# Waits, one store and the width of the output matmuls in a delta-rule attention and MLP kernel

## The reference

```python
k_n = k / (np.linalg.norm(k, axis=-1, keepdims=True) + 1e-06)
for t in range(S):
    y[:, :, t] = q_t @ state                  # per batch and head, state is D x D
    state = state + bt * outer(k_t, v_t - state.T @ k_t)
x = y.transpose(0, 2, 1, 3).reshape(B * S, H * D)          # 3072 x 384
x = ((x @ w1) * (x @ w2) @ w3) @ w_out                     # 384 -> 1024 -> 1024 -> 384
h = x @ w_in;  solu = h * softmax(h)
out = layernorm(solu) * g_ln @ w_out2                      # 3072 x 384
```

## Time and profile before

| | us |
|---|---|
| median of 3 runs | 771.3 (770.77 to 774.82) |
| the profiled execution | 769.96 |
| its span | 768.2 |
| PE busy | 742.0 (97%) |
| DVE busy | 455.4 (59%) |
| ACT busy | 340.2 (44%) |
| POOL busy | 61.6 (8%) |

### The profile page before, as it was taken

How to read it: one execution, slowest core, us unless ns; L and a number is a source line. 1 busy time by engine, 2 the same in 40 slices (tenths; PEclk the granted TensorE clock), 3 DMA queues, 4 the chain that set the end, 5 groups by cost and what they waited for, 6 DMA issues and landing times.

```text
span 768.2 us, 22375 instructions
## 1 busy us (share of the span) xinstructions
PE 742.0 (97%) x9652; PEld 667.7 (87%) x9652; DVE 455.4 (59%) x759; ACT 340.2 (44%) x704; POOL 61.6 (8%) x97
## 2 busy tenths in 40 slices
PE   7999899999999999999999899999999999999995
PEld 5667898998998999899999888888899999999985
DVE  2956965882894786489221644533456666666662
ACT  5646246236345424623424434433444444444442
POOL 2424100100000010010000000000000000000000
PEclk9999999999999999999999999999999999999998
DMA  9970350341044035031113475620000000000000
GB/s 268 337 229 15 111 170 31 75 148 51 30 121 124 30 88 171 30 93 56 44 40 124 130 235 174 192 76 1 10 22 22 20 20 20 20 21 22 23 18 31
DMA packets 38279, 66.16 MB, mean 86 GB/s; under 512 B 3568, under 2 KB 26224, under 8 KB 38192
## 3 DMA queue, kind: packets, MB, share of 16 engines
q1 hardware_dynamic: 35312, 58.34, 25.2%
q10 hardware_dynamic: 2880, 6.52, 2.6%
HBM read 45.98 MB, written 18.87 MB: 84 GB/s over the span
## 4 chain that ended last, share of the span: by engine, by line
PE 87%; ACT 5%; DMA 3%; DVE 3%; issue 1%; ACTq 0%; DVEq 0%
PE ps L1483 26%; PE ps L535 13%; PE ps L499 13%; PE ps L512 12%; PE ps L1496 4%; PE ps L1442 3%; PE ps L1399 3%; PE ps L524 3%; PE ps L1365 3%; PE ps L1453 3%; ACT gd L1190 2%; DMA mfirst<-in_wo 2%; PE ps L1416 2%; PE ps L1428 1%; PE ps L1357 1%
## 5 line engine op out<-in xcount | busy, mean ns | idle before, releaser
L1073 DVE TENSOR_TENSOR msb<-asb,ps 128x256 f32<-128x256 f32 x96 | 40.1, 417 | 113.3 <-ACT asb L1258 108.1
L1258 ACT COPY asb<-ps 128x256 f32<-128x256 f32 x96 | 35.7, 372 | 159.8 <-PE ps L1483 159.4
L535 PE MATMUL ps<-woh,uth 128*128 128x384 f32 x192 | 64.7, 337 | 0.5 <-DVE utl L452 0.5
L535 PE MATMUL ps<-woh,utl 128*128 128x384 f32 x192 | 64.5, 336 | 0.0
L535 PE MATMUL ps<-wol,uth 128*128 128x384 f32 x192 | 64.3, 335 | 0.0
L1483 PE MATMUL ps<-xh,w1h 128*128 128x256 f32 x288 | 57.4, 308 | 4.8 <-DVE msb L1073 4.8
L452 DVE TENSOR_TENSOR utl<-ps,uth 128x512 fp32r<-128x512 f32 x48 | 31.1, 686 | 48.2 <-ACT uth L342 48.2
L328 ACT ACTIVATE e<-ps,stats 128x1024 f32<-128x1024 f32 x24 | 26.8, 1116 | 67.3 <-DVE stats L418 67.3
L499 PE MATMUL ps<-mh,w34h 128*128 128x512 f32 x144 | 56.0, 389 | 0.0
L499 PE MATMUL ps<-ml,w34h 128*128 128x512 f32 x144 | 56.0, 389 | 0.0
L499 PE MATMUL ps<-mh,w34l 128*128 128x512 f32 x144 | 56.0, 389 | 0.0
(11 more groups left out here) (161 smaller groups left out, 1631.0 us busy)
## 6 DMA issues: line engine op xcount, KB each, us to landing
m_dram<-msb SPq DMA_DIRECT2D x42, 256.0 KB, 2.3
mrest<-m_dram SPq DMA_DIRECT2D x36, 256.0 KB, 5.6
vs<-in_vtok SPq DMA_DIRECT2D x6, 768.0 KB, 8.8
out<-wst SPq DMA_DIRECT2D x24, 192.0 KB
kt<-in_keys SPq DMA_DIRECT2D x22, 192.0 KB, 5.4
ks<-in_ktok SPq DMA_DIRECT2D x5, 768.0 KB, 5.2
mfirst<-m_dram SPq DMA_DIRECT2D x12, 256.0 KB, 5.4
z<-in_queries SPq DMA_DIRECT2D x10, 256.0 KB, 6.8
```

The costliest lines, as they stand in the source:

```text
L535: ins = pe.matmul(ob[s], xx[:, j, k, :], w[:, 4 * j + k, :], start=(j == 0 and k == 0 and p == 0), stop=(j == 1 and k == 3 and p == 2))
L1073: dve.tensor_tensor(msb[:, f // 2 % 2, f % 2, :], asb[:, f % 2, :], bbank[f % 2], ALU.mult).then_inc(product, 1)
L1258: act.copy(asb[:, f % 2, :], abank[f % 2]).then_inc(a_kept, 1)
```

## The change

Seven edits:

1. SP waits for the second half of wo1 (wo1_in[1]) ahead of its two first query loads.
2. In group 0 DVE does product_of(1, 1), the first product of all, ahead of below_first instead of behind it.
3. On ACT, keep_gram of tile 1 moves behind keep_u and a_of(1), for all groups.
4. The products f = 4 to 7 of the last half (11) go into rr and ysb (`stage`) instead of msb, DVE does not wait for m_sent ahead of them, and the stores read from there.
5. Since rr's and ysb's memory is later used by the MLP stage, ACT waits for all m_sent ahead of its first hh copies.
6. `outputs` splits each matmul of 64 stationary columns into two of 32.
7. Each output store becomes two of 64 rows, and the waits on o_sent count twice as far.

```diff
@@ mlp_programs, sync @@
-                    sp.dma_start(out_rows[2 * g:2 * g + 2, bass.ds(C * chunk, C), :],
-                                 osb[:, g, :]).then_inc(o_sent[g], 16)
+                    for bb in range(2):
+                        sp.dma_start(out_rows[2 * g + bb, bass.ds(C * chunk, C), :],
+                                     osb[64 * bb:64 * (bb + 1), g, :]).then_inc(o_sent[g], 16)
             for j in range(2):
-                sp.wait_ge(o_sent[j], 16 * NT // 2)
+                sp.wait_ge(o_sent[j], 2 * 16 * NT // 2)
@@ mlp_programs, scalar @@
-                    act.wait_ge(o_sent[s], 16 * sent)
+                    act.wait_ge(o_sent[s], 2 * 16 * sent)
...
                     act.wait_ge(h2_kept, KD * (NG - 2))
+                    for j in range(2):
+                        act.wait_ge(m_sent[j], 16 * 2 * 2 * NG)
                     high_h(0, 0)
@@ attention_programs @@
+        def stage(half, f):
+
+            if half == 2 * NG - 1 and f >= KF // 2:
+                t = (rr, ysb)[f // 2 % 2]
+                return t[:, :, :].rearrange("p g n -> p (g n)")[:, 0:2 * HT].rearrange("p (f c) -> p f c", f=2)
+            return msb[:, f // 2 % 2, :, :]
...
-                sp.dma_start(m_dram[half, :, f:f + 2, :], msb[:, f // 2 % 2, :, :]).then_inc(m_sent[f // 2 % 2], 16)
+                sp.dma_start(m_dram[half, :, f:f + 2, :], stage(half, f)).then_inc(m_sent[f // 2 % 2], 16)
@@ sync @@
             load_w3(1)
+            sp.wait_ge(wo1_in[1], 16)
             for tt in range(2):
                 first_queries(tt)
@@ vector, multiply @@
-                if f % 2 == 0 and not static_below(half, 1) or f >= 4:
+                if half == 2 * NG - 1 and f >= KF // 2:
+                    pass
+                elif f % 2 == 0 and not static_below(half, 1) or f >= 4:
                     dve.wait_ge(m_sent[f // 2 % 2], 16 * (2 * half + f // 4))
                 elif f == 0:
                     dve.wait_ge(w_low, 2 * KF)
-                dve.tensor_tensor(msb[:, f // 2 % 2, f % 2, :], asb[:, f % 2, :], bbank[f % 2],
+                dve.tensor_tensor(stage(half, f)[:, f % 2, :], asb[:, f % 2, :], bbank[f % 2],
                                   ALU.mult).then_inc(product, 1)
@@ vector, group @@
                     keep_pt(n + 1, nxt, NP, gbank[0])
+                if n == 0:
+                    product_of(1, 1)
                 if ahead:
                     below_first(n + 1, EB, EB, 0)
-                product_of(1, 1)
+                if n > 0:
+                    product_of(1, 1)
                 right_hand2(n, 1)
@@ scalar, group @@
                     if early and n > 0:
-                        for tile in range(NP):
-                            keep_gram(n + 1, tile)
+                        keep_gram(n + 1, 0)
                     keep_u(q, 0, u1_done, u1_kept)
                     if early and n == 0:
-                        for tile in range(NP):
-                            keep_gram(n + 1, tile)
+                        keep_gram(n + 1, 0)
                     a_of(1)
+                    if early:
+                        keep_gram(n + 1, 1)
                     if early:
                         keep_gram(n + 1, 2)
@@ tensor, outputs @@
-                        ins = pe.matmul(chain[g][u_rows(bb), hc(h)], z[r, par, bb, tile, h, :],
-                                        us[r, g, bb, hc(h)], start=True, stop=True)
+                        for half in range(2):
+                            at = HB * half
+                            ins = pe.matmul(chain[g][64 * bb + at:64 * bb + at + HB, hc(h)],
+                                            z[r, par, bb, tile, h, at:at + HB],
+                                            us[r, g, bb, hc(h)], start=True, stop=True)
```

More of the change, by code:

```diff
@@ L1262, in send_m @@
                 act.wait_ge(product, KF * half + f + 2)
-                act.dma_start(m_dram[half, :, f:f + 2, :], msb[:, f // 2 % 2, :, :]).then_inc(m_sent[f // 2 % 2], 16)
+                act.dma_start(m_dram[half, :, f:f + 2, :], stage(half, f)).then_inc(m_sent[f // 2 % 2], 16)
             def group(n, ahead):
```

## The result

The changed kernel takes 763.55 us (median of 9 runs, 759.38 to 767.29) beside 771.3 us (767.55 to 774.82). The ratio is 0.9891, 95% interval 0.986 to 0.9922, so the change gives 8.4 us (6.0 to 10.8); the forecast was 13.0 us. The profiled execution has a span of 761.8 us, against 768.2. I show first what the new trace has at each place that the prediction named.

The account below looks back on a forecast made before the run. TensorE, busy 97% of the span, was taken to bound the kernel. Gains of 2.6 + 1.4 + 4.0 + 0 + 1.2 + 3.8 = 13.0 us off 771.3 us gave 758.3 us, range 750 to 766 us.

Parts of the forecast that it names:

- What bounds the kernel: Whole span: TensorE busy 97%; time counts only where PE stands still, its blocks get shorter, or in the tail.
- Part 1: Start: SP's wait for wo1's second half ahead of the first queries saves 2.6 us, bounds -1 and 3.5.
- nothing gained: Lower bound at the start, -1 us: the w3 piece for f = 2 lands late and takes the gain back.
- Part 2: Group 0, second half: first product ahead of one DVE pair saves 1.4 us, bounds 0 and 2.9.
- Part 3: Groups 1 to 4: second gram copy behind keep_u removes cross blocks' waits for ACT, 4.0 us, bounds 2.5 and 4.5.
- Part 4: Last half's products f = 4 to 7 into rr and ysb: wait for m_dram stays, 0 us; other end 2.1.
- Rival (d): The staging also removes the m_dram wait at 424 us; 756.2 us, chance 0.06.
- Part 5: Outputs by 32 columns: blocks save 5.7 us, instruction stops cost 4.5; net gain 1.2 us, bounds 5.7 and -3.
- rival (c): Outputs: matmuls sharing rows overlap only two deep, so blocks get longer; 783 us, chance 0.09.
- Part 6: Tail: output stores as two of 64 rows shorten the last landing, saving 3.8 us, bounds 2.5 and 4.3.
- Rival (b): Start and group 0 give nothing: withheld loads or the next DVE step take both back; 762.3 us, chance 0.15.
- Rival (a): Outputs: the instructions come in time, so the split saves the full 5.7 us; 753.8 us, chance 0.20.

Follow-up runs that it names:

- b2_gate: Kernel before the change plus only SP's wait for the second half of wo1 ahead of the first queries; -0.3 us (-1.8 to +1.2).
- c3_group0: Kernel before the change plus only group 0's product_of(1, 1) moved ahead of below_first on DVE; -0.2 us (-1.8 to +1.2).
- a2_no_outputs: Changed kernel with the matmuls of outputs whole again, all other edits kept; ratio 0.9869 to the kernel before, -10.1 us.
- a4_stage_first: Changed kernel, but the last half's products f = 0 to 3 go to rr/ysb instead of f = 4 to 7; 761.55 us, ratio 0.9872.
- a1_outputs: Kernel before the change plus only the split of each outputs matmul into two of 32 columns; +2.9 us (+1.4 to +4.4).
- b1_stores: Kernel before the change plus output stores as two of 64 rows, with o_sent waits counting twice as far; -3.3 us (-4.8 to -1.8).
- a3_fill_between: Changed kernel with the MLP block of slot 5 between the two tiles' outputs and add_state instead of behind them; 759.53 us, ratio 0.985.

## Why the prediction was off, step by step

**What bounds the kernel.** Held: each gain appeared where PE stopped standing still, in its shorter blocks or in the tail.

**Part 1, start (taken 2.6, alone 0.3 us; at most 1.8).** This step failed. The gate opened when I had said (SP issues its query loads at 14.54 us and the piece for f = 2 at 15.37) and the piece landed at 15.37 + 7.3 = 22.7 us in the change, against my 21 to 22; in b2_gate at 16.13 + 9.0 = 25.1. My lower bound, "up to 1 us given back", left out that waiting again drops the clock: in b2_gate 3.18 us of wait are followed by 8 records that take 5.49 us instead of about 2.8. The end called "nothing gained" was the case. The next limit was misplaced as well. The sum let at most 2.65 us pass the w3 piece f = 6; in the change PE was 2.0 us ahead at 48.6 us, and there a packet of instructions took all of it, a term that the sum did not have.

**Part 2, group 0 (taken 1.4, alone 0.2 us, with 1.4 still inside the interval).** The two successors came as named, the right-hand side and the second product, and the stretch got 1.5 us shorter in the trace of c3_group0. But what shrank was not the waiting: the two waits sum to 2.68 us against 2.81, as the prediction's "about 1 and 2 us" already implied. The 1.4 us sat in the dates that I subtracted (92.4 less 91.0), and the first of these carries the slow records behind the old wait, which the sum does not name. By their starts the six groups behind the wait took 3.6 us before and 2.3 us behind the second wait in c3_group0, so the gain is the clock that stayed up. Where it falls, as in a2_no_outputs, little is left: my bound of 0 had said so. In the changed kernel itself the stop of 2.13 us in the cross block stands where the wait was, the clock falls behind it, and from the first outputs to those of the second half it is 27.7 us, against 27.8 before and 26.4 in c3_group0.

**Part 3, gram copies (taken 4.0, alone 4.9 us).** Held, in mechanism and size.

**Part 4, m_dram (taken 0).** Held: the wait is still there at 4.3 us, and a4_stage_first showed why, since swapping the two halves of the products removes it. Rival (d) fell.

**Part 5, outputs (taken +1.2, alone -2.9 us).** The mechanism was right and the size was wrong. The blocks gave 0.25 us each, as forecast, so rival (c) fell. The rule of the Trainium skill, TensorE: Matmul & The Clock Gate, section "Wait — 56ns, not 53.3ns?", that starts never come closer than about 25 ns, does not hold here: 64 records in 0.82 us are 12.8 ns each. The term mis-sized is the stops: 4.5 us more than before were taken, and from 60 us on it was 8.6 us in a1_outputs and 7.4 in the change. Two things were missing. The stops from 90 us on were nine, more than half of eleven stretches, and by the starts of the records they were 0.6 to 1.3 us long, 1.0 on average instead of 0.8. And one of 2.1 us fell into the cross block of group 0, a stretch that I had not priced at all since its instructions did not change: but every packet's edge behind a longer stream falls elsewhere. That one was free in a1_outputs, where PE had stood there for DVE anyway, and in the change it took what part 2 would have won. The lower bound of -3 us, with 9 us of stops, is the value that came; that it came so closely is in part luck, since the sum has neither the free stop nor the 1.9 us of slower up projections in a1_outputs. By "mostly hidden" of the Trainium skill, Runtime: NRT & Kernel Launch, section Instruction fetch mechanics, this part would have gained 5.7 us; a1_outputs measured a loss.

**Part 6, stores (taken 3.8, alone 3.3 us).** Held in mechanism and, within the interval, in size. The prediction's own figures, 2.8 instead of 6.1 us, give 3.3 and not the 3.8 that it took. In the traces of b1_stores and of the change the stretch behind the last matmul is 4.1 us shorter.

**The sum.** The two traces are 6.4 us apart, and this is where: the first outputs start 1.5 us later, the stretch to the outputs of the second half is 0.2 us shorter, that from there to the MLP stage 3.6 us, and the tail behind the last matmul 4.1 us. The five parts measured alone give -0.3 - 0.2 - 4.9 + 2.9 - 3.3 = -5.8 us, each with about 1.5 us of uncertainty, and together they give -8.4 (-10.8 to -6.0); the two agree within that. My sum was 13.0: parts 1, 2 and 5 were too high by 2.3, 1.2 and 4.1 us, parts 3 and 6 together too low by 0.4. That leaves 2.6 us by which the whole is better than its parts, which the intervals cover and no run explains; that the forecast ended within 5.3 us of the measurement owes something to it. Rival (b), given 0.15, is what happened to parts 1 and 2, and its 762.3 us lies nearer to the measured 763.6 than the forecast does. Rival (a) fell with the new stops.

## What to carry to other kernels

- A shorter block on the bounding engine is only a gain if its instructions still arrive: count the instructions of the densest stretch and its time. Here a stretch of 384 in 3.3 us stopped where a packet's edge fell into its later part, and with 3 us of long matmuls in the middle the split is worth 4.4 of its 5.5 us.
- When a wait is removed by holding back other loads, price the next wait with the clock's fall behind it, and not by the missing microseconds of the landing alone.
- Where one engine's chain sets the pace of a stretch, exchanging two of its steps only splits the other engine's wait in two; what it can still save is the clock's fall behind a long wait.

## What the runs showed of the hardware

- **Instruction supply.** 10420 matmuls and 10420 weight loads for 77 packets of 16 KB are 271 a packet. Each of the eleven stops of the change ends 2.3 to 2.7 us after such a packet starts, for instance at 162.86 us after one that started at about 160.6 us. Stops of 0.6 to 1.3 us fell in dense stretches; the two longest of the change, 2.53 and 2.13 us, came at 51 and 86 us, and the first of them came with whole outputs too. A float32 matmul counts four instructions: 64 of them shift the stream by a whole packet and leave ten of eleven stops on their record (58 and 6 of 64), 32 move them all.
- **The granted clock after a wait.** In a2_no_outputs PE stood 1.9 us for the product that waits for m_dram, and the windows behind it read

```profile
425.00:427.00 2.00, 2.00 (x11) 2.00 (x12) 2.00 (x3) 0.00 (x0) 0.00 (x0) 0.58 0.06 23
427.00:429.00 2.00, 2.00 (x13) 2.00 (x12) 0.15 (x1) 0.22 (x1) 0.00 (x0) 0.57 0.32 117
```

  with a granted clock (third column from the end) of 0.58 and 0.57, mostly the level of 1.2 GHz, while after waits of 2.0, 1.3 and 1.6 us at the same place in the traces of before, the change and a3_fill_between it stayed at 1.00. What tips it is open. Such dips go with part of the scatter between executions of one kernel: those of the change had a mean granted clock of 0.993 at 767.29 us and 0.998 at 759.38 us.
- **Concurrent matmuls that share their rows** go at the pace of those that share none: 0.82 us for 64 records of 112 or 128 rows by 32 columns, 0.81 us for 64 of 32 by 32.
- **The shape of a store.** 192 KB in one store with a leading dimension of 2 kept SP waiting 6.1 us; two stores of 96 KB with 64 leading land in 2.1 us each.
